# Second batch's gate moved into the last attention steps, with 16-column stationary weights

## The reference

```python
# 1: attention with 4 sink keys and a window of 128
a = softmax(where(is_sink | in_window, q @ k.T / 8, -1e9)); attn = a @ v
x = attn.transpose(0, 2, 1, 3).reshape(1536, 512)
# 2: mixture of 8 experts, each takes exactly 192 tokens
logits = x @ w_gate                       # 1536 x 8
# all (token, expert) pairs in descending order of logit: a token goes to the
# first expert that still has room
out[tokens of e] = relu(x[tokens of e] @ w1[e]) @ w2[e]     # 512 -> 1024 -> 512
# 3: gated product
y = ((out @ w_a) * (out @ w_b)) @ w_out   # 512 -> 1536 -> 512
```

## Time and profile before

| | |
|---|---|
| median of 3 executions | 690.67 us (690.64 to 693.61) |
| profiled execution, its time | 689.06 us |
| its span | 687.3 us |
| TensorE busy | 622.6 us, 91% of the span |
| VectorE busy | 328.6 us, 48% |
| ScalarE busy | 301.5 us, 44% |
| GpSimd busy | 136.8 us, 20% |
| mean granted TensorE clock | 0.939 of full |

### The profile page before, as it was taken

How to read it: one execution, slowest core, us unless ns; L and a number is a source line. 1 busy time by engine, 2 the same in 40 slices (tenths; PEclk the granted TensorE clock), 3 DMA queues, 4 the chain that set the end, 5 groups by cost and what they waited for, 6 DMA issues and landing times.

```text
span 687.3 us, 10549 instructions
## 1 busy us (share of the span) xinstructions
PE 622.6 (91%) x3666; PEld 529.3 (77%) x3666; DVE 328.6 (48%) x979; ACT 301.5 (44%) x685; POOL 136.8 (20%) x74
## 2 busy tenths in 40 slices
PE   7999999999212699999999999999999999999995
PEld 4877776788111699999999888888888888888884
DVE  4677656761886187777777522212221213222221
ACT  3676665660000177777777433323342415141411
POOL 3000000000000602222222005050613223441402
PEclk8999999996555699999999999999999999999999
DMA  9954150220300636766676505050604131523001
GB/s 191 265 130 92 48 169 24 85 87 23 122 0 3 184 95 214 233 207 233 244 229 199 184 0 184 0 184 2 242 17 166 51 132 61 183 73 110 0 0 61
DMA packets 85812, 81.22 MB, mean 118 GB/s; under 512 B 39697, under 2 KB 62225, under 8 KB 85777
## 3 DMA queue, kind: packets, MB, share of 16 engines
q1 hardware_dynamic: 83856, 74.49, 36.2%
q0 software_dynamic: 1920, 6.29, 2.7%
HBM read 74.48 MB, written 6.29 MB: 118 GB/s over the span
## 4 chain that ended last, share of the span: by engine, by line
PE 85%; DVE 8%; issue 2%; ACT 2%; POOL 1%; DMA 1%; DVEq 0%; ACTq 0%; POOLq 0%
PE psum L1406 15%; PE psum L1399 15%; PE psum L1400 14%; PE psum L1401 14%; PE psum L1407 7%; PE psum L1244 5%; PE psum L1222 3%; PE psum L1209 3%; PE psum L1249 2%; DVE above L938 2%; PE psum L1186 2%; PE psum L1258 1%; PE psum L1276 1%; PE psum L1390 1%; PE psum L1282 1%
## 5 line engine op out<-in xcount | busy, mean ns | idle before, releaser
L498 POOL TENSOR_TENSOR w_lo<-w_raw,w_hi 128x2048 fp32r<-128x2048 f32 x23 | 106.5, 4646 | 298.3 <-ACT w_hi L575 298.3
L575 ACT ACTIVATE w_hi<-w_raw 128x1024 fp32r<-128x1024 f32 (+1 forms) x126 | 123.5, 999 | 18.7 <-PE psum L1401 18.7
L1150 DVE TENSOR_TENSOR g_sb<-psum,a_sb 128x512 f32<-128x512 f32 x36 | 24.9, 692 | 197.0 <-PE psum L1401 197.0
L1399 PE MATMUL psum<-y_hi,w_hi 128*128 x288 | 113.1, 393 | 0.0
L1401 PE MATMUL psum<-y_hi,w_lo 128*128 x288 | 112.2, 389 | 0.0
L1400 PE MATMUL psum<-y_lo,w_hi 128*128 x288 | 112.1, 389 | 0.0
L735 DVE TENSOR_TENSOR w_lo<-w_raw,w_hi 128x1024 fp32r<-128x1024 f32 x64 | 77.8, 1215 | 0.0
L1406 PE MATMUL psum<-x_hl,w_hi 128*128 (+1 forms) x256 | 75.2, 365 | 1.6 <-DVE x_hl L1100 1.6
L1406 PE MATMUL psum<-h_hl,w_hi 128*128 128x384 f32 x256 | 74.6, 361 | 0.0
L1407 PE MATMUL psum<-x_hl,w_lo 128*128 (+1 forms) x256 | 64.7, 253 | 0.0
L1399 PEld LDWEIGHTS psum<-y_hi,w_hi 128*128 128x128 f32 x288 | 54.0, 188 | 13.5 <-POOL w_lo L498 2.5
(11 more groups left out here) (154 smaller groups left out, 998.3 us busy)
## 6 DMA issues: line engine op xcount, KB each, us to landing
w_raw<-in_moe_w_dram SPq DMA_DIRECT2D x32, 1024.0 KB, 5.1
w_raw<-in_moe_w_a_dram SPq DMA_DIRECT2D x9, 1024.0 KB, 5.2
w_raw<-in_moe_w_b_dram SPq DMA_DIRECT2D x9, 1024.0 KB, 5.1
w_raw<-in_moe_w_out_dram SPq DMA_DIRECT2D x9, 1024.0 KB, 5.5
k_raw<-in_k_dram SPq DMA_DIRECT2D x16, 192.0 KB, 3.8
q_raw<-in_q_dram SPq DMA_DIRECT2D x16, 192.0 KB, 4.0
v_sb<-in_v_dram SPq DMA_DIRECT2D x16, 192.0 KB, 4.2
xs_scratch<-x_rows SPq DMA_DIRECT2D x8, 384.0 KB, 3.6
```

Source lines behind the costliest of these rows:

```text
L498: nc.gpsimd.tensor_tensor(ring_lo[u][:, :], raw[u][:, :], ring[u][:, :].bitcast(f32), ALU.subtract).then_inc(w_lo[u], 1)
L575: op = nc.scalar.activation(ring[slot][:, ps], raw[r][:, ps], ACT.Copy)
L1150: nc.vector.tensor_tensor(g_sb[:, j % 2, :], bank[2 + j % 2][:, :], a_sb[:, j % 2, :], ALU.mult).then_inc(g_prod, 1)
L1399: nc.tensor.matmul(o, lhs_hi, rhs_hi, start=first, stop=False)
```

## The change

The second batch's gate is done by products with `wg` stationary, as in the first batch, one at a time in the steps from 44 on, except for its last piece.

- `wg` becomes `[P, KD, 3, E]`: the weights stand in the middle of three groups of 8 columns, with zeros left and right. A slice of 16 columns is then "weights, zeros" for the first half of the tokens and "zeros, weights" for the second, and both halves add into one 16x384 region of bank 7 (`last_gate`). Seven of the eight products of (half, block) are done so. `LAST_GATE` places them: steps 44, 45 and 46 have two each (blocks 0, 1, 2), step 47 one (first half, block 3).
- The "direct" jobs are gone. The "rows" jobs of the last pair write banks 0 and 1 (`rows_bank`), because bank 7 holds the sums meanwhile.
- VectorE copies the 16x384 sums to a new tile `LT2` after step 47. After the loop TensorE turns them to tokens (three products of 128x16 into bank 2), waits for the last "rows" copy, and adds the eighth piece by token, three products of 128x8. VectorE copies 128x48 logits at once and starts routing after a wait for its own copy.
- GpSimd clears `wg` first (a memset of 128x96), and SyncE loads it after that.
- GpSimd's and VectorE's start of routing waits for `gate_ready`.

The core of the diff:

```diff
-        wg = sb("wg", [P, KD, E], stack=attn)
+        wg = sb("wg", [P, KD, 3, E], stack=attn)
+        LT2 = sb("LT2", [2 * E, S // 2], stack=attn)
...
-            return sorted(jobs) + [(STEPS_A - 1, 1, "direct", last, 0), (STEPS_A, 1, "rows", last, 1),
-                                   (STEPS_A, 1, "direct", last, 1)]
+            return sorted(jobs + [(STEPS_A, 1, "rows", last, 1)])
...
+        LAST_GATE = {(STEPS_A - 4, 0): (0, 0), (STEPS_A - 4, 1): (1, 0), (STEPS_A - 3, 0): (0, 1),
+                     (STEPS_A - 3, 1): (1, 1), (STEPS_A - 2, 0): (0, 2), (STEPS_A - 2, 1): (1, 2),
+                     (STEPS_A - 1, 1): (0, KD - 1)}
+
+        def rows_bank(g, half):
+            return half if g == PAIRS - 1 else 7
...
-                    sp.dma_start(wg[:], w_gate.rearrange("(t p) e -> p t e", p=P)).then_inc(wg_in, 16)
                     sp.wait_ge(consts, 2)
+                    sp.dma_start(wg[:, :, 1, :], w_gate.rearrange("(t p) e -> p t e", p=P)).then_inc(wg_in, 16)
...
+            nc.gpsimd.memset(wg[:], 0.0)
...
-            pool.wait_ge(side_done, SIDES)
+            pool.wait_ge(gate_ready, 1)
...
+                if t == STEPS_A - 1:
+                    dve.wait_ge(gate_sums, 1)
+                    nc.vector.tensor_copy(LT2[:], bank[7][0:2 * E, 0:HS]).then_inc(sums_kept, 1)
...
-            dve.wait_ge(side_done, SIDES)
+            dve.wait_ge(gate_ready, 1)
+            nc.vector.tensor_copy(L[:, NCH - NBLK:NCH, :].rearrange("p (z i) e -> p z i e", z=2),
+                                  bank[2][:, 0:NBLK * E].rearrange("p (i z e) -> p z i e", z=2, e=E)
+                                  ).then_inc(logits_kept, 1)
+            dve.wait_ge(logits_kept, 1)
...
-            def direct(half, blocks):
-
-                for t in blocks:
-                    for i in range(3):
-                        at = (3 * half + i) * P
-                        op = nc.tensor.matmul(bank[half][:, i * E:(i + 1) * E], xT[:, t, at:at + P], wg[:, t, :],
-                                              start=(t == 0 and i == 0), stop=(t == KD - 1), skip_group_check=True)
-                return op
+            def last_gate(half, blk):
+
+                both = wg[:, blk, 1 - half:3 - half, :].rearrange("p z e -> p (z e)")
+                return nc.tensor.matmul(bank[7][0:2 * E, 0:HS], both, xT[:, blk, half * HS:(half + 1) * HS],
+                                        start=(half == 0 and blk == 0), stop=(blk == KD - 1))
...
+                if (t, late) in LAST_GATE:
+                    half, blk = LAST_GATE[t, late]
+                    pe.wait_ge(side_done, side_number("rows", PAIRS - 1 if blk == KD - 1 else PAIRS - 2,
+                                                      0 if blk == KD - 1 else 1) + 1)
+                    op = last_gate(half, blk)
+                    if blk == KD - 1:
+                        op.then_inc(gate_sums, 1)
...
+            pe.wait_ge(sums_kept, 1)
+            for i in range(3):
+                nc.tensor.matmul(bank[2][:, 2 * E * i:2 * E * (i + 1)], LT2[:, i * P:(i + 1) * P],
+                                 ident[0:2 * E, 0:2 * E], start=(i == 0), stop=False, skip_group_check=True)
+            pe.wait_ge(side_done, SIDES)
+            for i in range(3):
+                last = nc.tensor.matmul(bank[2][:, 2 * E * i + E:2 * E * (i + 1)],
+                                        xT[:, KD - 1, HS + i * P:HS + (i + 1) * P], wg[:, KD - 1, 1, :], start=False,
+                                        stop=True, skip_group_check=True)
+            last.then_inc(gate_ready, 1)
```

More of the change, by code:

```diff
@@ L215, in attention_moe_gated_product_kernel @@
         x_kept = sem("x_kept")
+        gate_sums = sem("gate_sums")
+        sums_kept = sem("sums_kept")
+        gate_ready = sem("gate_ready")
+        logits_kept = sem("logits_kept")
         dve_step = sem("dve_step")
@@ L622, in side_jobs @@
                     else:
-                        nc.scalar.activation(xT[:, g % NPAIR, half * HS:(half + 1) * HS], bank[7][:, 0:HS],
-                                             ACT.Copy).then_inc(side_done, 1)
+                        nc.scalar.activation(xT[:, g % NPAIR, half * HS:(half + 1) * HS],
+                                             bank[rows_bank(g, half)][:, 0:HS], ACT.Copy).then_inc(side_done, 1)
             def round_ahead(t):
@@ L816, in side_jobs @@
                     else:
-                        src = bank[half] if kind == "direct" else bank[7]
-                        nc.vector.tensor_copy(L[:, c0:c0 + 3, :], src[:, 0:3 * E].rearrange("p (i e) -> p i e", e=E)
+                        nc.vector.tensor_copy(L[:, c0:c0 + 3, :], bank[7][:, 0:3 * E].rearrange("p (i e) -> p i e", e=E)
                                               ).then_inc(side_done, 1)
@@ L1275, in side_jobs @@
                         for i in range(3):
-                            op = nc.tensor.transpose(bank[7][:, i * P:(i + 1) * P],
+                            op = nc.tensor.transpose(bank[rows_bank(g, half)][:, i * P:(i + 1) * P],
                                                      x_rows[:, b * NBLK + 3 * half + i, pr * P:(pr + 1) * P], ident[:])
@@ L1281, in side_jobs @@
                         for blk in range(KD):
-                            op = nc.tensor.matmul(bank[7][0:E, 0:HS], wg[:, blk, :], xT[:, blk, hs], start=(blk == 0),
+                            op = nc.tensor.matmul(bank[7][0:E, 0:HS], wg[:, blk, 1, :], xT[:, blk, hs], start=(blk == 0),
                                                   stop=(blk == KD - 1))
@@ L1287, in side_jobs @@
                                                      LT[:, half * HS + i * P:half * HS + (i + 1) * P], ident[0:E, 0:E])
-                    elif kind == "direct":
-                        op = direct(half, range(KD) if half == 0 else range(KD - 1, KD))
                     else:
@@ L1294, in side_jobs @@
                     op.then_inc(side_ready, 1)
-                    if kind == "direct" and half == 0:
-                        direct(1, range(KD - 1))
+                if (t, late) in LAST_GATE:
[5 more added lines that the diff above has]
+                        op.then_inc(gate_sums, 1)
             pe.wait_ge(spin_ready, 1)
```

## The result

| | median of all executions | range |
|---|---|---|
| kernel before | 693.4 us (20) | 690.57 to 702.66 |
| changed kernel | 690.0 us (20) | 687.08 to 698.7 |

The ratio is 0.9948, 95% interval 0.9926 to 0.9971: about 3.6 us faster, somewhere between 2 and 5. The gain that was forecast, 3.9 us, lies between 2 and 5; the measured time, 690.0 us, lies outside the predicted range of 684.3 to 689.6. The kernel before is itself 2.7 us slower by 20 executions than by the three that the prediction started from: two of those three (690.64 and 690.67) are among the five lowest of the 20.

What follows compares the result with a forecast made beforehand. TensorE bounds the path from turn 44 to the last `values`, with half clock from 159.1 us. The tail's 14.11 us becomes 9.59, 4.5 less; minus 0.6 for the experts gives 3.9, so 690.67 becomes 686.8 us, range 684.3 to 689.6.

Steps and rivals of the forecast that it cites:

- I predict against the median: 690.67 - 3.9: Whole kernel: median of the runs shown, 690.67 us, less the gain of 3.9 us, gives 686.8 us; chance 0.62.
- Of the stretch it wanted 4.5 us: From the end of `values(46)` to the sum of |L|: 9.59 us instead of 14.11, 4.5 us less.
- 0.6 us had been taken off for the experts: At the experts' start: a later clock rise could cost 1.2 us; half of that, 0.6 us, was allowed.
- I take 0.67: Turns 44 to 47: each 16-column gate product costs 0.67 us as in the first batch, seven 4.69 us.
- They stand on the path: Turns 44 to 47: no other engine's wait hides the gate products, so nothing below 4.69 us is possible.
- 0.34 us for three of 8 rows: Turn to tokens behind the last transposes: 0.34 us, 0.60 at half clock, against TensorE's wait of 0.55 there.
- I let it fall 1.5 us behind the last `values`: Tail: the clock falls as the three last products are issued, so they take 1.48 us instead of 0.85.
- the first rival: Tail: half clock once `values(47)` is through, transposes 0.91 us instead of 0.55, time 687.1 us; chance 0.15.
- dear gate products: Turns 44 to 47: gate products cost 0.82 us each, gain 2.8 us, time 687.9 us; chance 0.06.
- No fall of the clock in the gate turns: Slower rival: strewn narrow gate products pull the clock down from turn 44, time 698.1 us; chance 0.05.
- none right behind the last gate product: Rival: half clock from the last gate product's end, `values(47)` 1.1 us longer, time 688.2 us; chance 0.09.
- The experts moved with the start of routing: Experts: an earlier routing start passes through whole; the rival of no effect, 690.7 us, had chance 0.03.

Runs made afterwards that it cites:

- j_wide_row: Kernel before's 21 direct products in a row behind `values(46)`, streaming 64 columns instead of 8, with the changed kernel's `wg` setup: 689.76 us, ratio 0.9952 to kernel before.
- b: Changed kernel with all seven 16-column gate products in a row behind `values(46)` instead of strewn over four turns: 688.16 us, ratio 0.9906 to kernel before.
- e_single: Changed kernel with the turn of `LT2` to tokens made by one-pass transposes into three banks: 690.1 us, ratio 0.9946 to kernel before.
- n_fill_after: Changed kernel plus nine filler products at the start, where TensorE waits for the first exponentials: 684.98 us, ratio 0.9909 to kernel before.
- d_spin: Changed kernel plus ten filler products ahead of the first turn of gathered rows at the experts: 690.17 us, ratio 0.9957 to kernel before.

## Why the prediction was right and wrong

**The level was wrong, and with it the range.** The step that failed is "I predict against the median: 690.67 - 3.9". Three executions were taken for the level. By 20 it is 693.4, and 693.4 - 3.9 = 689.5 would have been within 0.5 us of the 690.0 measured. The prediction itself noted that the three spread by 3 us "which fits a clock that rises and falls at other moments each time", and then gave that spread no room: the range had bounds for the tail and the experts and none for the start, where the earlier trace rows showed 5.8 us of half clock from the first product on (6.8 with the wait ahead of it). The traces show 13.6, 6.8 and none at that place, and single dents of 3.4 us inside attention, of which the first trace of the kernel before has none. The mean granted clock says the same of the level: the profiled execution had 0.939, 26 executions of the kernel before 0.9335 on average.

**The gain was right, in part by luck:** 3.9 us forecast, 3.4 by the medians, 3.6 by the ratio. Of the stretch it wanted 4.5 us, and the traces give 3.6 on average; the net came out so near because 0.6 us had been taken off for the experts, where the average rise of three traces each (4.1 and 5.0 us behind their first product) makes 0.4 us. What the parts outside the stretch add or take, the dents above all, was in no term of the sum.

**Direct products and clock: right, and the main thing.** The prediction read half clock in the 7.75 us of 21 narrow products, and said that what follows them pays too. j_wide_row shows it. What I could not tell from one trace is that the fall 1.5 us into the row was one draw: it was 2.4 and 0.3 us in two others.

**Gate products: mis-sized.** "I take 0.67" was for products in a row. Alone they measured 0.75, halfway to the upper bound of 0.82: 5.2 us instead of 4.69, 0.5 us lost. That the clock would hold was right in all four traces of the changed kernel's gate turns, and so was "They stand on the path": b shows no gain from their places.

**The turn to tokens: mis-sized, and its cover was gone.** "0.34 us for three of 8 rows", at half clock 0.60. That row was of transposes, one pass each (x3); the change uses plain products, two passes (x6), as its diff says. They took 0.77 us at full clock and 1.39 at half, where 0.55 was covered, and held up the last products by 0.2 and 0.8 us. e_single shows the second: without it the stretch is 0.7 us shorter, the products taking 1.46 us there for 1.39.

**When the clock falls in the tail:** I let it fall 1.5 us behind the last `values`. It fell 0.4 us behind them in one trace, at 168.9, and 2.7 us behind them in another, at 170.8; in n_fill_after it was 0.5 and in d_spin 3.7. So the forecast and the first rival (half clock directly behind `values(47)`) are not two theories of which one is true but two draws. The rule that the Trainium skill gives in "TensorE: Matmul & The Clock Gate", section "Part 4: PE-mode transpose", would have the transposes of the tail at half clock; the second trace has them at 0.52 us, full clock, and the first at 0.87. It decides nothing here.

**The experts' rise:** 0.6 us was allowed for. It came 3.1 us after the first product in the first trace of the kernel before, 4.9 in its second, and 4.7, 5.4 and 4.9 in three of the changed kernel. By the first trace alone the change seemed to lose 0.7 us there; against the second, nothing.

**The other rivals:** dear gate products happened by half (0.5 of 1.06 us). No fall of the clock in the gate turns, and none right behind the last gate product: `values(47)` took 1.03 us in all four traces. The experts moved with the start of routing: 59.4 us from the sum of |L| to their first product before and after (171.75 to 231.12, 172.99 to 232.43).

## What to carry to other kernels

Where the page shows a half clock, ask first what a change does to the clock, and only then count instructions: here the same 21 products with a wider stream gained as much as the whole rewrite. Before forecasting a time, and not only a difference, look at how far executions of the same kernel lie apart and which stretches at half clock could make that; then compare traces by a stretch that starts and ends at the same work, because the whole span of one trace can say the opposite of the times; and look at the mean clock of all executions, which shows whether the traced one is like the rest. A price from a row in the trace holds for the same kind of instruction in the same company: one pass or two, in a row or alone.

## What the hardware showed that was not expected

- Three fp32 products with 128x128 stationary weights took 0.77 us at full clock with 8 streamed columns and 0.81 with 64 (strewn; in a row 0.69 with 64), so the wider stream was nearly free, while the clock fell in the one case and not in the other.
- A 16x384 fp32 product cost 0.75 us alone among other shapes and 0.66 in a row.
- 4.43 us of bf16 fillers in a row at half clock did not bring the clock up, while with nine fillers at the start it was up there in all three traces, and without them in one of eleven.
- The changed kernel has dents of half clock inside attention work that looks the same in every turn, 3.4 us long in the changed kernel's first trace (148.4 to 151.8), at other places in others.
